# Complex mixing by three real products for two groups at a time, inverse by halves of the array

## The chip, the cores and the metric

The kernel runs on one core of a Trainium2 chip. The metric is the time of one execution on the device in microseconds; the median of three runs before the change is 1173.78 us (1173.12 to 1173.87). The chip has a matrix engine (TensorE: PE for its products, PEld for its weight loads), a vector engine (VectorE, DVE), a scalar engine (ScalarE, ACT), GpSimd (POOL) and a queue engine that only issues transfers (SyncE, SP). They run side by side, each in the order of its own program, and meet at semaphores. Products are written to eight banks of PSUM, of 512 fp32 columns each.

## What is computed

A Fourier layer over a sequence of 3008 tokens (2 sequences, 256 channels), and two feed-forward layers behind it:

```python
X = np.fft.rfft(x, axis=1)
Xr, Xi = (X.real.astype(np.float32), X.imag.astype(np.float32))
Yr = Xr @ w_r - Xi @ w_i + b_r
Yi = Xr @ w_i + Xi @ w_r + b_i
lam = 0.01
Yr = np.sign(Yr) * np.maximum(np.abs(Yr) - lam, 0.0)
Yi = np.sign(Yi) * np.maximum(np.abs(Yi) - lam, 0.0)
y = np.fft.irfft(Yr + 1j * Yi, n=x.shape[1], axis=1)
h = y @ w_in_1;   g = relu(h) + alpha * min(h, 0);            y = g @ w_out_1
h = y @ w_in_2;   g = piecewise quadratic of h;               y = g @ w_out_2
```

The change is in the mixing (the lines of Yr and Yi), in the threshold behind it and in the first step of the inverse transform.

## The kernel before

**The transform.** 3008 is 47 times 64. A first product over 47 points (`real47`, 16 tiles of x) is stored to DRAM and read back in another order (tile `zt`, a quad of four groups, 2 transfers for each quad). Then come 48 steps, one for each group of 64 frequencies (24 groups in each of 2 sequences). A step `s` on TensorE is, in program order: `forward(s)` (the 64-point transform, two fp32 products of 128 columns into `xt_bank[s % 2]`), now and then two late tiles of `real47`, `mix(s - 1)` (12 products of 256 columns into `y_bank`) and `inverse(s - 2)` (one fp32 product of 256 columns into `v_bank`). Two groups share a pair of matrices (`gc`, read from DRAM for each pair) and a pair of results (`v_sb`, stored to DRAM for each pair).

**What the mixing multiplies.** Numbers are split into a high and a low part (f32r), and each product is done as high by high, high by low and low by high. So a step has 2 halves of the channels, 2 parts (real and imaginary) and 3 such terms: 12 products. ScalarE writes the high parts (`split_xt`, L644, L645, the second with the sign turned), VectorE the low parts (L887, L889).

**The threshold** is three operations of VectorE (`threshold`: bias added, L899; clipped, L902; the clipped value taken away, L907). ScalarE's `take_v` (L653) brings the inverse out of PSUM.

**The order around it.** Each engine's order is written out by hand. SyncE's queue holds, for each pair `p` from 3 on: `load_matrices(p)` (L359), for even `p` `load_values(p // 2)` (L370: the quad `zt` that forward of the pair `p` reads), loads of weights (L387, L389), and `store_pair(p - 3)` (L381), which waits for `take_v` of both groups of pair `p - 3`. So the quad that pair `p` reads is issued behind the store of pair `p - 4`. There are two buffers of `zt`.

**Jobs at the end of the transform.** From step 36 on the first tokens of the feed-forward layer are made: `tokens(0, job)` (TensorE, L1187, jobs 0 to 3 at steps 36, 38, 40 and 44), each into the one bank `side_bank`; the next may begin only when ScalarE (`side_copy`, `side_hi`) and VectorE (`side_lo`, `side_t1` and so on) have read the bank (`side_free`). They do that at the end of their steps 37, 39 and 41 to 43.

**The feed-forward layers** (from 153 us on) are products of 376 columns by a seven-product scheme (L1202) and their output products (L1294). The change doesn't touch them.

Of the kernel before, what the change touches and what calls it, by code (L numbers as in the profile page):

```python
# [5 lines left out]
P = 128  # L6
# [27 lines left out]
LATE_TILES = {1: (9,), 3: (10, 11), 5: (12, 13), 7: (14, 15)}  # L34
LATE_STORES = {n: (t, part) for n, (b, part, t) in enumerate(
    (b, part, b * TILES_PER_BATCH + t) for b in range(BATCH) for part in range(1 - b, STORE_PARTS)
    for t in range(0, TILES_PER_BATCH, 2))}
# [5 lines left out]
WAIT_PRODUCTS = {TILES_PER_BATCH - 1: 4 * (512,), TILES_PER_BATCH: 2 * (512,)}  # L43

CLIP_STEPS = WEIGHT_STEP = 21
# [5 lines left out]
SLOTS = 3  # L51

# [19 lines left out]
TOKEN_STEPS = {36: 0, 38: 1, 40: 2, 44: 3}  # L72
# [13 lines left out]
def transform_constants():  # L86
# [39 lines left out]
    both = np.stack([fwd_g, inv_g], axis=2).reshape(GROUPS // 2, 2, P, 2 * P)  # L126
    pairs = both.transpose(0, 2, 1, 3)
    return fwd.astype(np.float32), inv.astype(np.float32), pairs.reshape(GROUPS // 2, P, 4 * P).astype(np.float32)
# [12 lines left out]


def step_pair(s):

    return (s // 2) % SLOTS, (s // 2) // SLOTS


def fft_mix_ffn_kernel(nc, x, wmix, bias, alpha, wpack, fwd47, inv_in, group_consts, out):
# [16 lines left out]
    with ctx:  # L165
# [21 lines left out]
        half = sb("half", [P, 1])  # L187
        ut = [sb(f"ut{i}", [P, TILE_COLS]) for i in range(2)]
# [6 lines left out]
        wm_hi = sb("wm_hi", [P, 4 * D], f32r, fft)  # L195
        wm_lo = sb("wm_lo", [P, 4 * D], f32r, fft)
        bias_sb = sb("bias_sb", [P, D], scope=fft)
        xt_hi = [sb(f"xt_hi{i}", [P, DC, 3 * N2], f32r, fft) for i in range(SLOTS)]
        xt_lo = [sb(f"xt_lo{i}", [P, DC, 3 * N2], f32r, fft) for i in range(SLOTS)]
        y_sum = sb("y_sum", [P, D], scope=fft)  # L200
        y_clip = sb("y_clip", [P, D], scope=fft)
        y_out = [sb(f"y_out{i}", [P, D], scope=fft) for i in range(SLOTS)]
        raw_in_sb = [sb(f"raw_in_sb{i}", [P, (W + 1) * P], scope=fft) for i in range(RAW_SLOTS)]
        raw_out_sb = [sb(f"raw_out_sb{i}", [P, 2 * D], scope=fft) for i in range(RAW_SLOTS)]
        wm_raw = sb("wm_raw", [P, 4 * D], scope=fft)
# [19 lines left out]
        v_bank, xt_bank, y_bank = bank[2], bank[4:6], bank[7]  # L225
        clip_bank = bank[3]
        late_banks = ((bank[0], bank[1]), (bank[3], bank[6]))
# [9 lines left out]
        idle_ready = sem("idle_ready")  # L237
        wm_hi_ready = sem("wm_hi_ready")
# [11 lines left out]
        xt_hi_ready = sem("xt_hi_ready")  # L250
        xt_lo_ready = sem("xt_lo_ready")
        mix_done = sem("mix_done")
        y_sum_ready = sem("y_sum_ready")
        y_clip_ready = sem("y_clip_ready")
# [48 lines left out]
        block = ctx.enter_context(nc.Block())  # L303

# [50 lines left out]
        def _(sp):  # L355
            def load_matrices(p):
                if p >= GC_SLOTS:
                    sp.wait_ge(inv_done, 2 * (p - GC_SLOTS) + 2)
# [24 lines left out]
            def load_weights(n):  # L383
                if n >= RAW_SLOTS:
# [17 lines left out]
            sp.dma_start(wm_raw[:, :], wmix).then_inc(wm_in, 16)  # L402
# [4 lines left out]
            load_x(sp, 9)  # L407
            load_matrices(1)
            load_first_values(1)
            load_x(sp, 10)  # L410
            load_x(sp, 11)
            load_matrices(2)
            load_values(1)
            load_x(sp, 12)
            load_x(sp, 13)
            sp.dma_start(alpha_sb[:, :], alpha).then_inc(const_in, 16)
            sp.dma_start(inv47[:, :], inv_in).then_inc(const_in, 16)
            load_x(sp, 14)
            load_x(sp, 15)

            for p in range(SLOTS, PAIRS):
                load_matrices(p)
                if p % 2 == 0:
                    load_values(p // 2)
                if p == 18:
# [68 lines left out]
        def _(pool):  # L494
# [31 lines left out]
            for s in range(WEIGHT_STEP, STEPS):  # L526
# [7 lines left out]
                if s == 41:  # L534
                    token_lo(0, T1, r[1][:, :])
                if s == 43:
                    token_lo(0, T2, r[0][:, :])
                if s == 45:
# [856 lines left out]
```

## Time and profile before

| | |
|---|---|
| median of 3 runs | 1173.78 us |
| the profiled execution, its own time | 1173.06 us |
| its span, first to last instruction | 1171.3 us |
| TensorE busy | 1161.5 us, 99% of the span |
| VectorE, ScalarE, GpSimd busy | 75%, 73%, 58% |
| TensorE's first product of the layers' output (L1294) | at 153.14 us |
| granted clock of TensorE | 1.00 of full speed |

The span counts from the first to the last instruction; 1.8 us of the profiled execution's own time lie outside it. A busy share is over the whole span. The transform is the first 150 us, and in it each engine's share has to be read by itself.

### The profile page before, as it was taken

What the parts mean: (1) busy time and instruction counts of PE and PEld (TensorE: products, weight loads), DVE (VectorE), ACT (ScalarE), POOL (GpSimd) and SP (SyncE); (2) the same over time, 40 slices, a digit from 0 to 9 for tenths busy, and PEclk for the clock granted to TensorE, in tenths of its full rate; (3) what the DMA queues carried; (4) which work ended last, traced back from release to release, by engine and by line L of the source; (5) the groups of instructions that cost most, each with busy time, mean ns of one, the idle gap of its engine ahead of it and who ended that gap; (6) DMA issues with size and microseconds to landing.
All of it is one profiled execution on the core that took longest, in us unless ns stands there. A gap on an engine that the chain in (4) does not pass through costs nothing.

```text
span 1171.3 us, 21142 instructions
## 1 busy us (share of the span) xinstructions
PE 1161.5 (99%) x7024; PEld 1135.1 (97%) x7024; DVE 882.4 (75%) x1675; ACT 853.7 (73%) x1880; POOL 684.7 (58%) x714
## 2 busy tenths in 40 slices
PE   8999999999999999999999999999999999999998
PEld 3899999999999999999999999999999999999998
DVE  3777777777777777777777787878778787878776
ACT  3445577777676777767677788888888787878776
POOL 0027547567575767666556666665657565756554
PEclk9999999999999999999999999999999999999999
DMA  9898312012120201202004500000000000000000
GB/s 324 312 304 267 123 55 67 29 41 65 49 77 28 68 28 60 77 29 68 19 20 162 197 19 1 27 1 27 1 27 1 28 1 27 2 27 1 14 14 27
DMA packets 41164, 79.56 MB, mean 68 GB/s; under 512 B 4576, under 2 KB 21088, under 8 KB 40288
## 3 DMA queue, kind: packets, MB, share of 16 engines
q1 hardware_dynamic: 38752, 68.65, 17.7%
q10 hardware_dynamic: 2304, 9.56, 2.1%
q8 instruction: 56, 0.92, 0.3%
q14 instruction: 52, 0.43, 0.1%
HBM read 47.92 MB, written 30.28 MB: 67 GB/s over the span
## 4 chain that ended last, share of the span: by engine, by line
PE 98%; DMA 1%; DVE 0%; issue 0%; SPq 0%; ACT 0%; ACTq 0%
PE bank L1294 45%; PE bank L1202 40%; PE bank L1168 6%; PE bank L1187 2%; PE bank L1178 2%; PE bank L1153 2%; DMA x_sb<-x 1%; PE bank L1138 1%; PE bank L1124 0%; DVE g_sb L1004 0%; SPq L339 0%; DVE y_sum L899 0%; DVE a_sb L872 0%; DVE bank L989 0%; DVE y_tile L1026 0%
## 5 line engine op out<-in xcount | busy, mean ns | idle before, releaser
L547 POOL TENSOR_TENSOR g_lo<-g_sb,g_hi 128x376 fp32r<-128x376 f32 x510 | 506.4, 1004 | 361.5 <-ACT g_hi L803 360.7
L1294 PE MATMUL bank<-g_hi,w_out_hi 128*128 128x376 f32 x1024 | 342.8, 335 | 0.0
L1294 PE MATMUL bank<-g_hi,w_out_lo 128*128 128x376 f32 x1024 | 341.5, 333 | 0.0
L1202 PE MATMUL bank<-xc_hi,w_in_hi 128*128 128x376 f32 x896 | 302.4, 338 | 0.1
L1202 PE MATMUL bank<-xc_hi,w_in_lo 128*128 128x376 f32 x896 | 299.6, 334 | 0.0
L1202 PE MATMUL bank<-xc_lo,w_in_hi 128*128 128x376 f32 x896 | 299.0, 334 | 0.0
L803 ACT ACTIVATE g_hi<-g_sb 128x376 fp32r<-128x376 f32 x512 | 261.2, 510 | 45.7 <-DVE g_sb L1004 28.8
L1294 PE MATMUL bank<-g_lo,w_out_hi 128*128 128x376 f32 x1024 | 259.6, 334 | 0.0
L1294 PEld LDWEIGHTS bank<-g_hi,w_out_hi 128*128 128x128 f32 x1024 | 192.2, 188 | 0.6
L1294 PEld LDWEIGHTS bank<-g_hi,w_out_lo 128*128 128x128 f32 x1024 | 192.7, 188 | 0.0
L1294 PEld LDWEIGHTS bank<-g_lo,w_out_hi 128*128 128x128 f32 x1024 | 184.2, 188 | 0.0
L1202 PEld LDWEIGHTS bank<-xc_hi,w_in_hi 128*128 128x128 f32 x896 | 168.3, 188 | 0.8 <-DVE g_sb L1004 0.4
L1202 PEld LDWEIGHTS bank<-xc_hi,w_in_lo 128*128 128x128 f32 x896 | 168.5, 188 | 0.0
L1202 PEld LDWEIGHTS bank<-xc_lo,w_in_hi 128*128 128x128 f32 x896 | 168.4, 188 | 0.0
L792 ACT ACTIVATE act_a<-bank,half 128x376 f32<-128x376 f32 x192 | 109.1, 568 | 43.9 <-PE bank L1202 43.1
L794 ACT ACTIVATE act_a<-act_a 128x376 f32<-128x376 f32 x256 | 133.0, 519 | 8.1
L1004 DVE SCALAR_TENSOR_TENSOR g_sb<-bank,neg_alpha,g_sb 128x376 f32<-128x376 f32 x192 | 115.7, 603 | 3.1 <-ACT bank L788 2.9
L787 ACT ACTIVATE g_sb<-bank 128x376 f32<-128x376 f32 x192 | 91.9, 479 | 34.2 <-PE bank L1202 33.0
L977 DVE TENSOR_TENSOR partial<-u,bank 128x376 f32<-128x376 f32 x128 | 69.5, 543 | 59.9 <-PE bank L1202 58.9
L1008 DVE SCALAR_TENSOR_TENSOR g_sb<-bank,act_a 128x376 f32<-128x376 f32 x192 | 104.6, 545 | 4.8 <-ACT act_a L794 1.2
L984 DVE TENSOR_TENSOR h<-partial,bank 128x376 f32<-128x376 f32 x128 | 69.8, 545 | 41.5 <-PE bank L1202 41.3
L788 ACT ACTIVATE bank<-bank 128x376 f32<-128x376 f32 x192 | 92.1, 479 | 0.0
(84 smaller groups left out, 1511.9 us busy)
## 6 DMA issues: line engine op xcount, KB each, us to landing
gc<-group_consts SPq DMA_DIRECT2D x24, 256.0 KB, 4.4
slots_scratch<-a_sb ACTq DMA_DIRECT2D x24, 256.0 KB, 4.4
inverse_scratch<-v_sb SPq DMA_DIRECT2D x24, 256.0 KB, 3.0
ut<-inverse_scratch SPq DMA_DIRECT2D x16, 384.0 KB, 5.0
out<-y_tile SPq DMA_DIRECT2D x30, 188.0 KB, 1.9
zt<-slots_scratch SPq DMA_DIRECT2D x22, 256.0 KB, 4.1
x_sb<-x SPq DMA_DIRECT2D x10, 512.0 KB, 8.9
prep_raw<-wpack SPq DMA_DIRECT2D x16, 256.0 KB, 2.7
```

The lines of the kernel that those rows point to most:

```text
L547: pool.tensor_tensor(g_lo[kind][:, :], g_sb[n % 3][:, :], g_hi[kind][:, :].bitcast(f32), ALU.subtract)\
L787: act.activation(gg, h, ACT.Relu)
L788: act.activation(h, h, ACT.Relu, scale=-1.0).then_inc(act_done, 1)
L792: act.activation(a, h, ACT.Relu, bias=half[:, 0:1], scale=0.5).then_inc(root_ready, 1)
L794: act.activation(a, a, ACT.Square).then_inc(act_done, 1)
L803: act.activation(g_hi[kind][:, :], g_sb[n % 3][:, :], ACT.Copy).then_inc(hi_ready, 1)
L984: dve.tensor_tensor(h22[:, :], partial[:, :], c12_bank[:, 0:N], ALU.add).then_inc(h_ready[C22], 1)
L1004: dve.scalar_tensor_tensor(out=gg, in0=h_of(kind), scalar=neg_alpha[:, f:f + 1], in1=gg, op0=ALU.mult, op1=ALU.add).then_inc(g_ready, 1)
L1008: dve.scalar_tensor_tensor(out=gg, in0=h_of(kind), scalar=1.0, in1=a, op0=ALU.max, op1=ALU.min).then_inc(g_ready, 1)
L1168: last = pe.matmul(y_bank[:, 0:D], xs[s % SLOTS][:, c, at:at + P], ws[:, (part * DC + c) * D:(part * DC + c + 1) * D], start=n == 0, stop= ...
L1202: done = pe.matmul(bank_of[:, 0:N], w_part[:, fp, w * P:(w + 1) * P], x_part[q % 2][:, xs, :], start=first and n == 0, stop=last_one and n ...
L1294: last = pe.matmul(acc_bank[k][c][:, 0:N], w[:, fp, upper * D + c * P:upper * D + (c + 1) * P], g_part[kind][:, :], start=first and n == 0 ...
```

## The change

Steps become pairs: TensorE runs, for each pair `p`, `forward(p)`, `mix(p - 1)`, `inverse(p - 2)`, one late tile of `real47` (pairs 2 to 8), and a token job (pairs 18 to 21). With A = Xr + Xi, the mixing of both groups is three real products over a stationary operand that holds both groups' values: A by w_r (`X_SUM`, into `sum_bank`), Xi by -(w_r + w_i) (`X_IM`) and Xr by (w_i - w_r) (`X_RE`), both into `parts_bank`. Yr is the first sum and the second, Yi the first and the third. So a pair has 3 products, 2 halves of the channels and 3 terms: 18 products of 256 columns. The sum A is made by VectorE in PSUM from a copy of Xi that ScalarE makes. The threshold is, of y with bias: over = relu(y - lam) on ScalarE and min(y + lam, over) on VectorE. The matrices of the inverse are laid out so that the rows 0 to 63 hold one group and the rows 64 to 127 the other, and the inverse of a pair is four fp32 products of 64 rows each: two for real and imaginary part of each group, one half of the array for each group, into two banks.

```diff
-LATE_TILES = {1: (9,), 3: (10, 11), 5: (12, 13), 7: (14, 15)}
+LATE_TILES = {2: 9, 3: 10, 4: 11, 5: 12, 6: 13, 7: 14, 8: 15}
-WAIT_PRODUCTS = {TILES_PER_BATCH - 1: 4 * (512,), TILES_PER_BATCH: 2 * (512,)}
+WAIT_PRODUCTS = 4 * (512,)
-TOKEN_STEPS = {36: 0, 38: 1, 40: 2, 44: 3}
+TOKEN_PAIRS = {18: 0, 19: 1, 20: 2, 21: 3}
...
@@ TensorE
-            def inverse(s):
-                matrices = gc[s // 2 % GC_SLOTS]
-                pe.wait_ge(y_ready, s + 1)
-                if s:
-                    pe.wait_ge(v_ready, s)
-                pe.matmul(v_bank[:, 0:D], matrices[:, (2 * (s % 2) + 1) * P:(2 * (s % 2) + 2) * P],
-                          y_out[s % SLOTS][:, :], start=True, stop=True).then_inc(inv_done, 1)
+            def inverse(p):
+                matrices = gc[p % GC_SLOTS]
+                pe.wait_ge(y_ready, p + 1)
+                if p:
+                    pe.wait_ge(v_ready, 2 * p)
+                for k in range(2):
+                    for g in range(2):
+                        rows = slice(N2 * g, N2 * (g + 1))
+                        last = pe.matmul(v_bank[g][:, 0:D], matrices[rows, (2 + k) * P:(3 + k) * P],
+                                         y_out[p % MIX_SLOTS][rows, k, :], start=k == 0, stop=k == 1)
+                last.then_inc(inv_done, 1)
+            for p in range(PAIRS):
+                forward(p)
+                if p == PAIRS - 1:
+                    make_p1(0)
+                if p:
+                    mix(p - 1)
+                if p == PAIRS - 1:
+                    side_free(0, 4)
+                    make_p6(0)
+                if p >= 2:
+                    inverse(p - 2)
+                if p in LATE_TILES:
+                    real47(LATE_TILES[p], late_bank, LATE_TILES[p])
+                if p in TOKEN_PAIRS:
+                    tokens(0, TOKEN_PAIRS[p])
@@ ScalarE
+            for p in range(PAIRS):
+                split_x(p)
+                split_sum(p)
+                for s in (2 * p, 2 * p + 1):
+                    weights_hi(s)
+                if p:
+                    over(p - 1)
+                if p == PAIRS - 1:
+                    take_p1(0)
+                if p >= 2:
+                    take_v(p - 2)
+                if p in LATE_TILES:
+                    copy_a(LATE_TILES[p], late_bank[0])
+                for s in (2 * p, 2 * p + 1):
+                    if s in LATE_STORES:
+                        store_a(act, *LATE_STORES[s])
+                if p == 19:
+                    side_copy(0, 0, r[0])
+                    side_hi(0, 0, B11)
+                if p == 20:
+                    side_copy(0, 1, r[2])
@@ VectorE
+            for p in range(PAIRS):
+                split_x(p)
+                sum_x(p)
+                if p:
+                    add_bias(p - 1)
+                    add_parts(p - 1)
+                split_sum(p)
+                if p:
+                    shrink(p - 1)
+                if p in LATE_TILES:
+                    copy_a(LATE_TILES[p], late_bank[1])
+                if p == 19:
+                    side_lo(0, 1, B11)
+                if p == 20:
+                    side_t1(0)
+                if p == 21:
+                    side_t2(0)
+                    side_lo(0, 2, B22)
+                    side_t3(0)
@@ SyncE: load_values keeps its place in the queue, and so does store_pair
-                    sp.wait_ge(b_done, 4 * (n - QUAD_SLOTS) + 4)
+                    sp.wait_ge(b_done, 2 * (n - QUAD_SLOTS) + 2)
```

**The first place: SyncE's queue around the quad of pair 8.** Before, the five transfers are the store of pair 4, the matrices of pair 8, its quad and the store of pair 5:

```order
L381 DMA inverse_scratch<-v_sb1 128x2x256 [waits v_ready]
L359 DMA gc0<-group_consts 128x512 [waits inv_done]
L370 DMA zt0<-slots_scratch2 64x4x256 [waits a_stored02,b_done]
L370 DMA zt0<-slots_scratch2 64x4x256
L381 DMA inverse_scratch<-v_sb2 128x2x256 [waits v_ready]
```

Of the changed kernel, the same stretch:

```order
L406 DMA inverse_scratch<-v_sb1 128x2x256 [waits v_ready]
L384 DMA gc0<-group_consts 128x512 [waits inv_done]
L395 DMA zt0<-slots_scratch2 64x4x256 [waits a_stored02,b_done]
L395 DMA zt0<-slots_scratch2 64x4x256
L406 DMA inverse_scratch<-v_sb2 128x2x256 [waits v_ready]
```

The queue's order is the same. What the store waits for (`v_ready` of pair 4) is what moves: TensorE's inverse of pair 4 was at steps 10 and 11, which is pair 5, and is now in pair 6.

**The second place: ScalarE in the pair 19, and what TensorE does there.** `xt_hi` and `x_im` are the split of the forward transform, `y_over` the threshold, `v_sb` the inverse of pair 17, and `r0` and `xc_hi0` read `side_bank` (bank 1) for the first token job. Before, from step 37 to step 38:

```order
L644 ACTIVATE xt_hi1<-bank5 128x2x128 [waits mix_done,b_done]
L645 ACTIVATE xt_hi1<-bank5 128x2x64
L653 ACTIVATE v_sb2<-bank2 128x256 [waits inv_done]
L662 ACTIVATE w_in_hi<-raw_in_sb2 128x896 [waits s_made]
L679 ACTIVATE r0<-bank1 128x376 [waits side_done]
L672 ACTIVATE xc_hi0<-bank1 128x376 [waits side_done]
L644 ACTIVATE xt_hi2<-bank4 128x2x128 [waits mix_done,b_done]
L645 ACTIVATE xt_hi2<-bank4 128x2x64
```

The changed kernel in pair 19:

```order
L668 ACTIVATE xt_hi1<-bank5 128x2x256 [waits mix_done,b_done]
L672 ACTIVATE x_im<-bank5 128x256 [waits x_sum_ready]
L676 ACTIVATE xt_hi1<-bank5 128x2x128 [waits x_sum_ready]
L704 ACTIVATE w_out_hi<-raw_out_sb2 128x512
L684 ACTIVATE y_over<-bank0,neg_lam 128x512 [waits y_ready,y_sum_ready]
L692 ACTIVATE v_sb2<-bank2 128x256 [waits v_stored2,inv_done]
L692 ACTIVATE v_sb2<-bank7 128x256
L718 ACTIVATE r0<-bank1 128x376 [waits side_done]
L711 ACTIVATE xc_hi0<-bank1 128x376 [waits side_done]
```

The two reads of bank 1 stand now behind `y_over`, which waits for VectorE's sum of this pair's mixing, and behind both halves of `v_sb`.

**The third place: TensorE at the end of the same pair 19**, from the inverse of pair 17 on:

```order
L1262 MATMUL bank2<-y_out1,gc1 128x256 [waits v_ready,y_ready]
L1262 MATMUL bank7<-y_out1,gc1 128x256
L1262 MATMUL bank2<-y_out1,gc1 128x256
L1262 MATMUL bank7<-y_out1,gc1 128x256
L1272 MATMUL bank1<-inv47_sb,ut1 128x94 [waits side_taken,t_made,b_lo_ready,u_in1]
L1272 MATMUL bank1<-inv47_sb,ut1 128x94 x3
L1227 MATMUL bank4<-gc0,zt0 128x2x64 [waits sum_lo_ready,gc_in0,zt_in0]
L1227 MATMUL bank4<-gc0,zt0 128x2x64 x3
```

Before, at step 38 (the first row is the inverse of step 36):

```order
L1178 MATMUL bank2<-y_out0,gc2 128x256 [waits v_ready,y_ready]
L1187 MATMUL bank1<-inv47_sb,ut1 128x94 [waits side_taken,t_made,b_lo_ready,u_in1]
L1187 MATMUL bank1<-inv47_sb,ut1 128x94 x3
L1153 MATMUL bank5<-gc3,zt1 128x128 [waits xt_lo_ready]
L1153 MATMUL bank5<-gc3,zt1 128x128
```

The second token job stood one step behind the step in which the other engines read bank 1 for the first; it stands now at the end of the same pair.

## Rows read from the trace of the kernel before

**Rows 1.** The page: busy time, and the chain that ended last.
```profile
PE 1161.5 (99%) x7024; PEld 1135.1 (97%) x7024; DVE 882.4 (75%) x1675; ACT 853.7 (73%) x1880; POOL 684.7 (58%) x714
PE 98%; DMA 1%; DVE 0%; issue 0%; SPq 0%; ACT 0%; ACTq 0%
```

**Rows 2.** Busy time by stretch: TensorE, VectorE, ScalarE, GpSimd; granted clock, DMA share.
```profile
0.00:20.00 20.00, 15.61 (x76) 4.59 (x76) 7.32 (x12) 7.42 (x12) 0.20 (x4) 1.00 0.89 336
60.00:100.00 40.00, 39.75 (x306) 38.33 (x306) 30.67 (x86) 19.31 (x58) 14.09 (x17) 1.00 0.85 283
```

**Rows 3.** The chain, 34 to 41 us: start, us, what.
```profile
34.74 1.43 PE bank L1168 x12
36.17 0.43 PE bank L1178 x2
36.60 0.44 PE bank L1153 x4
37.05 1.88 PE bank L1138 x16
38.92 1.62 PE bank L1168 x12
```

**Rows 4.** Timeline of TensorE in narrow windows: forward of pairs 0, 8 and 18; first L1294.
```profile
23.40 1.05 PE L1153 MATMUL bank<-gc,zt 128*128 128x128 f32 x8
65.96 0.38 PE L1153 MATMUL bank<-gc,zt 128*128 128x128 f32 x2
113.39 0.38 PE L1153 MATMUL bank<-gc,zt 128*128 128x128 f32 x2
153.14 0.34 PE L1294 MATMUL bank<-g_hi,w_out_hi 128*128 128x376 f32 x1
```

**Rows 5.** ScalarE behind a forward, twice; then groups of both engines by shape.
```profile
24.04 0.38 ACT L644 ACTIVATE xt_hi<-bank 128x256 fp32r<-128x256 f32 x1 [1.76 <-PE bank L1153]
66.78 0.39 ACT L644 ACTIVATE xt_hi<-bank 128x256 fp32r<-128x256 f32 x1 [0.23 <-PE bank L1153]
67.06 0.27 ACT L645 ACTIVATE xt_hi<-bank 128x128 fp32r<-128x128 f32 x1
L617 ACT ACTIVATE a_sb<-bank 128x512 f32<-128x512 f32 x16 | 9.6, 598 | 13.3 <-PE bank L1138 13.3
L880 DVE TENSOR_TENSOR wm_lo<-wm_raw,wm_hi 128x512 fp32r<-128x512 f32 x2 | 1.3, 688 | 1.9 <-ACT wm_hi L636 1.9
L887 DVE TENSOR_TENSOR xt_lo<-bank,xt_hi 128x256 fp32r<-128x256 f32 x48 | 20.3, 423 | 18.7 <-ACT xt_hi L645 17.7
L911 DVE TENSOR_TENSOR xc_lo<-bank,xc_hi 128x376 fp32r<-128x376 f32 x3 | 1.6, 546 | 1.1 <-ACT xc_hi L672 1.1
```

**Rows 6.** SyncE's queue: pair 4's store with the quad of pair 8; then pair 16's.
```profile
57.34 0.38 SPq L381 DMA_DIRECT2D inverse_scratch<-v_sb  x1
58.35 1.41 SPq L370 DMA_DIRECT2D zt<-slots_scratch  x2
113.99 0.38 SPq L381 DMA_DIRECT2D inverse_scratch<-v_sb  x1
```

**Rows 7.** The two issues of each of these quads, and their times to landing.
```profile
L370 SPq DMA_DIRECT2D zt<-slots_scratch x2: 675/684/692, 58.4 to 59.1; - x2
DMA to landing us min/median/max: 4.0/4.9/5.8
L370 SPq DMA_DIRECT2D zt<-slots_scratch x2: 591/604/617, 115.0 to 115.6; - x2
DMA to landing us min/median/max: 3.6/3.9/4.1
```

**Rows 8.** Timeline around the second token job, 120 to 123 us.
```profile
120.54 0.48 ACT L679 ACTIVATE r<-bank 128x376 f32<-128x376 f32 x1
120.90 0.49 ACT L672 ACTIVATE xc_hi<-bank 128x376 fp32r<-128x376 f32 x1
122.08 1.10 PE L1187 MATMUL bank<-inv_sb,ut 96*128 96x94 f32 x8 [0.39 <-issue]
```

More of the change, by code:

```diff
@@ L42 @@
 WARM_PRODUCTS = (512, 256)
[L43 to L45 removed]
+WAIT_PRODUCTS = 4 * (512,)
+WEIGHT_STEP = 21
+BANK_PAIRS = range(10, 21)
 FF = 2048
@@ L51 @@
 SLOTS = 3
+MIX_SLOTS = 2
+X_RE, X_IM, X_SUM = range(3)
 LAYERS = 2
@@ L836, in _ @@
                 prep_high(g)
+                if g == 0:
+                    over(PAIRS - 1)
+                    take_v(PAIRS - 2)
                 if g < ALL_GROUPS:
@@ L1094, in _ @@
                 if g == 0:
-                    threshold(STEPS - 1)
+                    add_bias(PAIRS - 1)
+                    add_parts(PAIRS - 1)
+                    shrink(PAIRS - 1)
                     dve.wait_ge(neg_ready, 1)
@@ L1140, in real47, with forward @@
                     last.then_inc(a_done, 1)
[L1142 to L1144 removed]
+            def forward(p):
+                quad, matrices = p // 2, gc[p % GC_SLOTS]
+                if p == 0:
                     pe.wait_ge(zt_first_in, 32)
[L1146 removed]
+                elif p % 2 == 0 or p == 1:
                     pe.wait_ge(zt_in[quad % QUAD_SLOTS], 32 * (quad // QUAD_SLOTS) + 32)
[L1148 to L1156 removed]
@@ new lines, in forward, with mix @@
+                for g in range(2):
+                    for c in range(DC):
+                        last = pe.matmul(xt_parts(p)[:, c, :, g, :],
+                                         zt[quad % QUAD_SLOTS][:, 2 * (p % 2) + g, c * P:(c + 1) * P],
+                                         matrices[:, g * P:(g + 1) * P], start=True, stop=True)
+                last.then_inc(b_done, 1)
+            def mix(p):
+                slot = p % MIX_SLOTS
+                for n, k in enumerate((X_IM, X_SUM, X_RE)):
+                    if p == 0:
+                        pe.wait_ge(wm_lo_ready, n + 1)
+                    if k == X_IM:
+                        pe.wait_ge(xt_lo_ready, p + 1)
+                        if p:
+                            pe.wait_ge(y_sum_ready, p)
+                    if k == X_SUM:
+                        pe.wait_ge(sum_lo_ready, p + 1)
+                    to = {X_IM: parts_bank[:, 0:D], X_SUM: sum_bank[:, 0:D], X_RE: parts_bank[:, D:]}[k]
+                    terms = [(c, xs, ws) for c in range(DC)
+                             for xs, ws in ((xt_hi, wm_hi), (xt_hi, wm_lo), (xt_lo, wm_hi))]
+                    for n, (c, xs, ws) in enumerate(terms):
+                        last = pe.matmul(to, xs[slot][:, c, k, :], ws[:, k, c * D:(c + 1) * D],
+                                         start=n == 0, stop=n == len(terms) - 1)
+                    if k == X_SUM:
+                        last.then_inc(sum_done, 1)
+                last.then_inc(mix_done, 1)
```

315 lines of the change are left out of this document (151 added, 164 removed).

## The prediction

> **What bounds the kernel now.** I read the page first: TensorE is busy 99% of the span and is 98% of the chain that ended last [rows 1]. A busy share is no proof by itself, so I read the transform by stretches: from 60 to 100 us TensorE works 39.75 of 40 us, VectorE 30.7 and ScalarE 19.3 [rows 2]. TensorE bounds each step, and the others have slack. The chain in order of time gives a step's parts: 12 mixing products 1.43 us (0.119 each), the inverse 0.43, the forward products 0.44, a step of 2.30 [rows 3]. Two late tiles take 1.88 us, and the mixing behind them 1.62 instead of 1.43. What the change does to time is then a question of two sums: how much of TensorE's work goes, and whether TensorE still finds its inputs ready. For the second I read SyncE's queue and how early each transfer lands.
>
> **The work that goes.** A pair has 18 mixing products for 24: 6 x 0.119 = 0.71 us, 17.1 us over 24 pairs. Two idle products go too (0.9 us, but they filled a wait). The forward products keep their columns.
>
> **The inverse by halves.** For a pair it is four fp32 products of 256 columns in place of two. If two halves run side by side, it takes the time of two, 0.86 us, as now. If they take turns, 1.72. The trace has no product of 64 by 128, but it has 64 by 64: sixteen records of 512 columns in 1.88 us [rows 3]. A record of the inverse with 256 columns takes 0.43 / 2 = 0.215 us; sixteen records of 512 in turn would take 16 x 0.43 = 6.9 us. So four run at a time, in both halves of the rows. I take side by side, and keep 0.86 us a pair for the range. There is a price for changing the array's shape: the two late tiles need 4 x 0.43 = 1.72 us and took 1.88, and the mixing behind took 0.19 more: 0.35 us for going in and out. Every pair goes in and out once now: 24 x 0.35 = 8.4 us, against four times before (1.4), and 7 more changes of shape between the inverse and a late tile (1.2). So TensorE's work falls by 17.1 + 0.9 - 8.4 + 1.4 - 1.2 = 9.8 us, and a pair without extras takes 0.88 + 2.14 + 0.86 + 0.35 = 4.2 us for 4.6 now. The Trainium skill, page "TensorEngine Tiling (Array Packing)", section "Tiling Modes", says that tiles work independently and that a change of the tiling mode drains TensorE; the 0.35 us agree with the second, and a sum without it would be 8.2 us better.
>
> **What a pair is waited for: the quad of `zt`.** The queue's order is unchanged: the quad that pair p reads is issued behind the store of pair p - 4, which waits for `take_v` of that pair. But the inverse of a pair now comes two pairs behind its forward, where it came two steps (one pair) behind. So the same transfers start a pair later while the reader stands where it stood. Today the slack is small: the store of pair 4 is issued at 57.34 [rows 6], the second half of the quad at 59.1 and it lands 5.8 us later [rows 7], at 64.9; the forward of pair 8 reads it at 65.96 [rows 4]. From store to landing: 7.6 us there, and 1.6 + 4.1 = 5.7 us for the store at 113.99 [rows 6, 7], when fewer transfers are under way. Moved by 4.2 us or more, the quad comes too late for each even pair.
>
> How long is the loop from one such forward to the next? From rows of the operations nearest in shape, counted from the forward's start:
> - ScalarE starts 0.64 us after four records of forward began (23.40 to 24.04) [rows 4, 5]; a pair has eight, so at 1.07. Its 512 columns take 0.60 [rows 5], and an independent operation starts 0.11 before the end of the last (66.78 and 0.39, then 67.06): `x_im` starts at 1.56 and ends at 1.95.
> - VectorE, 0.04 between dependent operations: low part 512 columns 0.69 to 2.68; `sum_x` 0.42 to 3.14; `add_bias` and `add_parts`, 0.69 each, start 0.08 before the last one's end: the second runs 3.67 to 4.36. The mixing of the pair before ended at 0.88 + 2.14 + 0.2 = 3.2, in time.
> - ScalarE: `over` from 4.40, 0.60; both `take_v` 0.39 each, to 5.56. The inverse has ended by then (4.2 + 0.2).
> - SyncE: the store at 5.6, and the next quad lands 5.7 to 7.6 later. Forward of pair p + 2 starts 11.3 to 13.2 us after that of pair p; now it is 9.2.
>
> I take 12.7 while late tiles and their stores load the DMA engines (they are busy 85% there [rows 2]) and 11.6 behind them. TensorE's wait is 2.5 to 3.5 us in each second pair. It is almost independent of what TensorE's own work costs: the loop doesn't pass through the inverse. That is why the saving of 0.4 us a pair is not added: it goes into the wait.
>
> **The token jobs.** Job 1 on TensorE now stands at the end of pair 19, and ScalarE and VectorE read bank 1 for job 0 only at the end of their own pair 19, behind `over` and `take_v`. Counted as above: `take_v` ends at 5.56, two reads of bank 1 (0.48, 0.49 [rows 8]) to 6.4, VectorE's low part 0.55 [rows 5] to 7.0. TensorE is there at 4.2 and waits 2.9 us; today it waits 0.39 [rows 8]. Job 2 waits for one read and one operation, some 2.7 us; job 3 for three operations of VectorE, 3.5. Pairs 18 to 22 take 5.1 + 8.0 + 7.6 + 8.3 = 29.0 us; a late quad hides behind these waits.
>
> **The sum, as a timeline of forward.** It starts at about 22.2 (23.40 now, for the two idle products less and the first values landing). The second half of the first quad is issued a transfer earlier, so pair 1 follows at 24.2. Then the pair's chain is bare: the mixing of pair 0 waits for VectorE's sum (0.6 us), that of pair 1 for the sum of pair 0 (1.2): pair 2 at 28.2, its store of pair 0 at 28.2 + 5.6 + 1.2 + 0.9 (two issues of ScalarE) = 35.9, the quad 7 us later: pair 4 at 43. Pair 10: 43 + 3 x 12.7 = 81. Pair 18: 81 + 4 x 11.6 = 127.5, for 113.39 now [rows 4]. Pair 22: 156.5. Pair 23: 160.7. From there to the first product of L1294 TensorE has forward 0.88, two mixings 4.28, three inverses 3.63, nine products of the layer at 3 x 0.119 x 376 / 256 = 0.52, 4.7, and one wait of 0.8 for the sum: 14.3 us. That is 175.0, for 153.14 now [rows 4]: **21.9 us later**. Nothing behind it changes, and TensorE is full there, so the end moves by the same. The profiled execution took 1173.06 us with a span of 1171.3; its span becomes 1193.2 and its time 1195.0. The median shown is 0.7 us above it, so I predict **1195.5 us**.
>
> **Rivals.**
> - *The quads arrive in time, and TensorE's own work decides* (0.05). It needs store to landing under 2 x 4.2 - 5.6 = 2.8 us; the two cases above are 5.7 and 7.6. Then pairs without late tiles take 4.2, those with one 5.2: pair 18 comes at 28 + 7 x 5.3 + 9 x 4.2 = 103; with 29.0 and 4.2 + 14.3 the first L1294 is at 150.5, 2.6 us earlier than now: 1171 us. This is the case on the other side.
> - *The halves take turns* (0.10). 0.86 us a pair more, of which the wait for the quad absorbs nearly all: `take_v` moves from 4.9 to 5.2, so 0.3 for each of 7 loops, 2.6 for the last three inverses, 1.5 at the start: 6 us more, 1201.5.
> - *The clock falls in the waits* (0.08). The longest stretches without work so far are at the start, where TensorE works 15.6 of 20 us and the granted clock stays 1.00 [rows 2]. Waits of 3 us in each second pair are new; if TensorE went to its lower level (1.2 in place of 2.4 GHz), the forward and mixing behind a wait, which do stand in the loop, would take up to 3 us more in up to ten loops: 1205 to 1225. The Trainium skill, page "TensorE: Matmul & The Clock Gate", section on why it matters for kernels, warns of idle gaps between bursts of products; no row here shows such a fall.
> - *The same mechanism, with lighter traffic* (0.09). With longer pairs there is less traffic, and if all quads took 5.0 us the loop would be 10.6: 7 loops save 1.0 to 2.1 each, 1186 or a little below.
>
> **How the numbers follow.** The forecast with its own range of 1187 to 1204 has 0.68. The range reaches down to the light traffic and up over halves in turn: 1185 to 1206, which leaves out the first rival and the clock. A measurement of this kernel can tell 0.2% (2.3 us) from no change. Slower: 0.94; the first rival splits into same (0.03) and faster (0.03).
>
> **What would show it.** In the changed profile: SyncE's store behind `take_v` and the quad landing just before forward of each even pair from 4 on; TensorE idle 2.5 to 3.5 us there, released by the transfer into `zt`; three waits of 2.7 to 3.5 us before L1272 in pairs 19 to 21; inverse records of both halves starting together, 0.86 us for a pair; 2.14 us for a pair's mixing; granted clock 1.00. The prediction is wrong if the wait before even pairs is under 1 us, if it is ScalarE's or VectorE's (the loop would then be longer in every pair), or if the clock falls.

## The result and the profile after the change

The changed kernel takes **1211.46 us** (median of 4 runs, 1208.11 to 1216.50), the kernel before 1173.49 (4 runs): ratio 1.033, 95% interval 1.029 to 1.037, so 38.0 us more where 22 more were forecast, and above the range. The four runs spread over 8.4 us, those of every other kernel here over 0.8 to 5.5 us; so a difference from this median of 1211.46 is known to some 5 us only. Two executions that ran at a granted clock of 0.75 all through (1399 us, the profiled one of e5_takes_early, and 1409 us, the kernel before) count in no comparison. The profiled execution is the longest of them: 1216.50 us, span 1214.7.

The page of the changed kernel first (L1227 is the forward, L1247 the mixing, L1262 the inverse, L1272 the token jobs, L1379 the output products; L1294 of the forecast is now L1379):

```profile
span 1214.7 us, 20878 instructions
PE 1169.0 (96%) x6972; PEld 1132.7 (93%) x6972; DVE 879.5 (72%) x1583; ACT 869.4 (72%) x1881; POOL 683.2 (56%) x714
PE   7877779999999999999999999999999999999998
PEclk8888889999999999999999999999999999999999
```

The reader is to see that nearly all the loss lies in the first six slices of 30 us, the transform (the first output product comes 42.1 us later than before, the end 43.4): there TensorE's busy digit falls to 7 and 8, and so does its granted clock, which the forecast had at 1.00. What TensorE waited for, in the view of its waits (us in total, times, longest):

```profile
PE bank L1227 <- DMA zt<-slots_scratch: 26.9, 10, 4.7
PE bank L1272 <- DVE xc_lo L981: 3.0, 1, 3.0
PE bank L1272 <- DVE r L998: 3.0, 1, 3.0
PE bank L1272 <- DVE r L989: 2.5, 1, 2.5
PE bank L1227 <- DMA gc<-group_consts: 0.8, 2, 0.5
```

These are the waits that were forecast, at the places that were forecast: `zt` before the forward of each even pair from 4 to 18, and three token jobs (2.9, 2.7 and 3.5 forecast). Two of the ten for `zt`, 1.1 and 1.4 us, stand before pairs 0 and 1. The other eight are 1.8 to 4.7 us long, 3.0 in the mean, where 2.5 to 3.5 was forecast. The stretches of 20 us answer to [rows 2] (TensorE's busy time in the second number, its granted clock third from the end):

```profile
20.00:40.00 20.00, 16.30 (x110) 13.64 (x110) 10.32 (x19) 7.60 (x17) 0.00 (x0) 0.83 0.75 261
60.00:80.00 20.00, 16.02 (x106) 13.21 (x107) 10.08 (x17) 8.12 (x20) 0.00 (x0) 0.83 0.67 234
80.00:100.00 20.00, 15.79 (x124) 12.73 (x122) 13.07 (x24) 10.00 (x23) 2.41 (x5) 1.00 0.68 225
140.00:160.00 20.00, 15.65 (x96) 14.60 (x97) 7.50 (x13) 7.56 (x17) 6.96 (x11) 0.76 0.59 183
```

A mean of 0.83 is a mixture of two levels, which short stretches behind a wait show apart:

```profile
35.00:42.00 7.00, 7.00 (x58) 4.78 (x58) 5.79 (x11) 3.28 (x8) 0.00 (x0) 1.00 0.53 167
46.00:51.00 5.00, 5.00 (x23) 5.00 (x24) 1.45 (x3) 1.25 (x3) 0.00 (x0) 0.50 0.86 334
63.00:68.00 5.00, 5.00 (x25) 4.84 (x23) 1.81 (x3) 1.25 (x3) 0.00 (x0) 0.50 0.62 214
82.00:87.00 5.00, 5.00 (x42) 3.79 (x34) 2.96 (x6) 2.82 (x7) 0.00 (x0) 1.00 0.64 210
```

From 46 to 51 us, right behind the wait for the quad of pair 4, TensorE is busy without a gap and gets 23 matmul records through; from 82 to 87 us 42. The one stretch is at 1.2 GHz, the other at 2.4. Single instructions show the same: a mixing product that starts each 0.12 us at full clock starts each 0.21 here.

```profile
41.27 1.09 PE L1212 MATMUL bank<-x_sb,fwd_sb 64*64 64x512 f32 x8
46.00 2.08 PE L1227 MATMUL bank<-gc,zt 128*128 128x128 f32 x8 [3.65 <-DMA zt<-slots_scratch]
48.09 0.41 PE L1247 MATMUL bank<-wm_lo,xt_hi 128*128 128x256 f32 x1
48.30 0.42 PE L1247 MATMUL bank<-wm_hi,xt_lo 128*128 128x256 f32 x1
...
51.23 0.28 PE L1247 MATMUL bank<-wm_lo,xt_hi 128*128 128x256 f32 x1
51.34 0.28 PE L1247 MATMUL bank<-wm_hi,xt_lo 128*128 128x256 f32 x1
```

The transform has eight such stretches, 41 us together; the first begins at 24 us, at the start, the other seven in or just behind one of the waits above. At most half of that, 20 us, is lost, less where the slower work lies in a wait.

The forward of pairs 0, 4, 10, 18, 22 and 23 starts at 23.3, 46.0, 89.9, 141.4, 176.3 and 180.6 us (forecast 22.2, 43, 81, 127.5, 156.5 and 160.7; before, [rows 4]), and the first output product at 195.2 (forecast 175.0).

One loop of the forecast, ScalarE, SyncE's queue and TensorE from 95 us on:

```profile
95.20 0.64 ACT L692 ACTIVATE v_sb<-bank 128x256 f32<-128x256 f32 x2
95.86 0.38 SPq L406 DMA_DIRECT2D inverse_scratch<-v_sb  x1
96.28 1.36 SPq L384 DMA_DIRECT2D gc<-group_consts  x1
97.74 1.25 SPq L395 DMA_DIRECT2D zt<-slots_scratch  x2
102.49 0.80 PE L1227 MATMUL bank<-gc,zt 128*128 128x128 f32 x2 [3.36 <-DMA zt<-slots_scratch]
```

The forward of pair 10 started at 89.91. `take_v` of its turn ends at 95.84, the store goes out at 95.86, 5.95 us behind the forward (5.6 forecast), the quad behind it is read at 102.49, 6.6 us later (5.7 to 7.6 forecast), and TensorE has waited 3.4 us.

### The profile page after: what moved, and what is told of

It is laid out like the page before. It is cut to its first block, busy times and chain, and to the rows that moved or that the text cites. A ratio compares the mean times of both kernels' runs of the same rounds, so it can differ in the third digit from the quotient of the medians.

```text
span 1214.7 us, 20878 instructions
## 1 busy us (share of the span) xinstructions
PE 1169.0 (96%) x6972; PEld 1132.7 (93%) x6972; DVE 879.5 (72%) x1583; ACT 869.4 (72%) x1881; POOL 683.2 (56%) x714
## 3 DMA queue, kind: packets, MB, share of 16 engines
q1 hardware_dynamic: 38752, 68.78, 17.1%
## 4 chain that ended last, share of the span: by engine, by line
PE 64%; DVE 0%; issue 0%
PE bank L1379 34%; PE bank L1287 29%; PE bank L1272 1%; DVE u L1044 0%; DVE y_tile L1098 0%
## 5 line engine op out<-in xcount | busy, mean ns | idle before, releaser
L1379 PE MATMUL bank<-g_hi,w_out_lo 128*128 128x376 f32 x1024 | 342.9, 335 | 0.0
L1379 PE MATMUL bank<-g_hi,w_out_hi 128*128 128x376 f32 x1024 | 342.4, 334 | 0.0
L1379 PE MATMUL bank<-g_lo,w_out_hi 128*128 128x376 f32 x1024 | 259.8, 335 | 0.0
L1379 PEld LDWEIGHTS bank<-g_hi,w_out_hi 128*128 128x128 f32 x1024 | 192.5, 188 | 0.8
L1379 PEld LDWEIGHTS bank<-g_hi,w_out_lo 128*128 128x128 f32 x1024 | 192.4, 188 | 0.0
L1379 PEld LDWEIGHTS bank<-g_lo,w_out_hi 128*128 128x128 f32 x1024 | 184.7, 188 | 0.0
```

The lines of the kernel that those rows point to most:

```text
L1379: last = pe.matmul(acc_bank[k][c][:, 0:N], w[:, fp, upper * D + c * P:upper * D + (c + 1) * P], g_part[kind][:, :], start=first and n == 0 ...
```

## The experiments

Each ratio is to the kernel before, timed on the same chip (its median was 1173.57 beside e1 to e4, 1174.47 beside e5 to e8, 1173.82 beside e9 to e11, 1174.35 beside e12); a difference between kernels of two of these groups carries that of the chips, up to 0.9 us.

**e1_quads_early** takes the quads' lateness away: SyncE issues the quad an iteration earlier, ahead of the store, and the store ahead of the late tile's x.

```diff
                 load_matrices(p)
-                if p % 2 == 0:
-                    load_values(p // 2)
+                if p % 2 and p + 1 < PAIRS:
+                    load_values((p + 1) // 2)
+                if p > SLOTS:
+                    store_pair(p - SLOTS - 1)
                 if p + 8 < TILES:
                     load_x(sp, p + 8)
...
-                store_pair(p - SLOTS)
```

> The changed kernel with one edit in SyncE's queue: the quad of pair p + 1 and the matrices of pair p are issued ahead of the store of pair p - 4, not behind it. Theory A (the waits for the quads, those of the token jobs, and a clock that falls in such waits): the ten waits for zt (26.9 us) go, and with them most falls of the clock; left are the three token waits (one of them longer, since a late quad no longer hides in it) and waits of 0.5 to 1 us per pair for VectorE's sum, because ScalarE's chain of a pair is 4.5 us and more. Time 1184 us (1179 to 1190). Rival B (the loop of ScalarE and VectorE is what limits a pair, the quad only happens to be last): the other waits take the place of these, 1200 us or more. Rival C (the clock falls for another reason, the 64-row products for one): still 6 to 8 falls, 1200 us.

Measured: 1193.66 us, ratio 1.017 (1.015 to 1.019), 17.8 us under the changed kernel and between theory A (1179 to 1190) and its rivals (1200). So the late quads, with what the clock does in their waits, were 17.8 of the 38 us. The wait for `zt` is 1.8 us in all, and other waits are longest:

```profile
PE bank L1273 <- DVE xc_lo L982: 4.5, 1, 4.5
PE bank L1273 <- DVE r L999: 3.6, 1, 3.6
PE bank L1228 <- issue: 3.5, 2, 3.0
PE bank L1248 <- DVE bank L969: 2.7, 4, 1.0
```

The token jobs' waits have grown, and the clock still fell four times, two of them there (120 to 140 us: 0.83, 140 to 160: 0.91).

**e2_quads_reads** is e1_quads_early and, on ScalarE and VectorE, the reads of bank 1 for the token jobs at the start of the next pair, ahead of that pair's own work.

```diff
 # ScalarE (VectorE alike, with side_lo, side_t1, side_t2, side_t3)
+                if p == 19:
+                    side_copy(0, 0, r[0])
+                    side_hi(0, 0, B11)
+                if p == 20:
+                    side_copy(0, 1, r[2])
...
-                if p == 19:
-                    side_copy(0, 0, r[0])
-                    side_hi(0, 0, B11)
```

> e1 with one more edit: ScalarE's and VectorE's reads of bank 1 for a token job stand at the start of the next pair, ahead of its split, not at the end behind y_over and v_sb. Theory A: the three token waits (8.5 us) nearly go, clock 1.00 throughout; ring waits for VectorE's sum remain. Time 1177 us (1173 to 1182), about 7 to 8 us below e1. Rival B: 1192 or more. Rival: VectorE is delayed by the reads at the start of the pair and gives the same back at the mixing: no better than e1.

Measured: 1181.25 us, ratio 1.007 (1.005 to 1.008): another 12.4 us, inside theory A's 1173 to 1182. **e9_reads_early**, run later, is the fourth corner: the reads moved by the same edit, the quads late as in the changed kernel.

> The changed kernel with its quads issued as they are, and only ScalarE's and VectorE's reads of bank 1 for token jobs 0 to 3 moved to the start of the pair that follows (so before that pair's own work instead of behind the pair's before). Theory A (the loop through the quad of zt sets the pace also in pairs 18 to 22, and the token waits lie beside it): 1 to 4 us off, 1209 (1206 to 1212). Theory B (the three token waits of 2.5 to 3.0 us stand in the sum on their own, and with them go two stretches at the half clock): 10 us off, 1201 (1198 to 1204).

Measured: 1197.36 us (1195.05 to 1200.38), ratio 1.020 (1.018 to 1.022), 14.1 below the changed kernel: theory A falls, and theory B's 1198 to 1204 is missed by a little. The token jobs' waits are gone, the quads' stay:

```profile
PE bank L1230 <- DMA zt<-slots_scratch: 23.6, 12, 4.0
```

Pairs 18 to 22 take 24.3 us for 34.9. So the four kernels read 1211.5 (neither), 1193.7 (quads), 1197.4 (reads), 1181.3 (both): the effects, 17.8 and 14.1, add up to the 30.2 of both within the spread of the runs. Two separate causes make four fifths of the loss; what the clock does in their waits is inside both.

How far one execution stands for a kernel shows here too. Up to pair 18 the program of e9_reads_early is that of the changed kernel, and its profiled execution is there at 130.96 us, the changed kernel's at 141.38. In the same 718 records of TensorE the one had a mean clock of 0.95, the other of 0.90:

```profile
0.00:130.70 130.70, 102.64 (x718) 76.93 (x718) 74.56 (x130) 61.62 (x134) 25.39 (x34) 0.95 0.76 256
0.00:141.00 141.00, 109.25 (x718) 81.72 (x718) 74.68 (x130) 61.93 (x134) 26.18 (x36) 0.90 0.71 237
```

**e3_fill_waits** asks what the clock costs: all waits stay, idle products stand in them (results unused), nine of 512 columns before the forward of the even pairs from 4 to 18, ten before token jobs 1 to 3.

```diff
+            def filler(p, n):
+                pe.wait_ge(sum_lo_ready, p - 1)
+                for _ in range(n):
+                    pe.matmul(xt_bank[p % 2][:, 0:512], wm_hi[:, 0, 0:P], wm_hi[:, 1, 0:512],
+                              start=True, stop=True)
...
+                if p >= 4 and p % 2 == 0 and p - 1 not in (19, 21):
+                    filler(p, 9)
```

> The changed kernel with products of no use (512 columns, f32r) ahead of the forward of the even pairs from 4 (9 products, 2.1 us) and ahead of token jobs 1 to 3 (10 products, 2.4 us), written to the bank that the next forward overwrites. All waits stay as late as they are, but TensorE works in them. If the waits make the clock fall (theory A): granted clock 1.00, and 1195 us (1191 to 1199), 16 us less than the changed kernel, which is the time that the late quads and tokens cost by themselves. If the clock falls for another reason: 1211 us and falls as before.

Measured: 1204.05 us (1203.29 to 1205.52), ratio 1.026 (1.025 to 1.028), between the two expectations (1195 and 1211). More work on TensorE, and 7.4 us less time: the reader should stop at that. All four runs lie below the changed kernel's fastest, 1208.11; by the spread of both, the 7.4 can be some 5 us more or less. Two stretches at the lower level are left, 10.2 us together, at 23.0 and 108.3 us:

```profile
20.00:40.00 20.00, 17.03 (x114) 14.22 (x116) 10.58 (x19) 7.61 (x17) 0.00 (x0) 0.83 0.76 265
40.00:60.00 20.00, 19.98 (x144) 14.97 (x140) 12.52 (x24) 9.04 (x21) 0.00 (x0) 1.00 0.92 310
```

They can cost 5.1 us at most. So of the 38 us the clock has 7.4 to 12.5, and without it the changed kernel would take 1199 to 1204. One run says more: the fastest of the four, 1203.29 us, had a mean granted clock of 1.000, so no such stretch, and is 0.8 us under the median. The clock's share is then near 8 us, and what the two stretches cost near 1. The idle products themselves hardly delay the quads: seven of the eight quads landed 0.04 to 0.05 us before the forward that reads them, the one of pair 6 half a microsecond before.

**e8_fill_all** was to close that gap: 13 and 12 products in place of 9 and 10, and four float32 products behind the ninth tile.

> The changed kernel with all its waits, and idle products in them: 13 before the forward of an even pair in place of the 9 of e3_fill_waits, 12 in place of 10 before the token jobs, and four more of 512 columns behind the ninth tile at the start. Theory A (the clock took about 10 us of the 38, the waits 28): the granted clock is 1.00 all through, the time 1200 us (1197 to 1203). Theory B (the idle products themselves delay the forward where they are longer than the wait): the clock is 1.00 and the time 1204 or more.

Measured: 1207.58 us, ratio 1.028 (1.027 to 1.030): theory B. The clock is 1.00 outside 20 to 40 us, and 1.000 in three of the four runs (1206.62 to 1207.94), but the products were longer than the waits. A float32 product of 512 columns is two records of 0.43 us, so the four take 3.4 us of the start at the full clock, and more where it is halved. It leaves the clock's share as it is.

**e4_before_late_quad** puts the suspected cost alone into the kernel before: its quad is issued behind the store of pair p - 3 instead of p - 4.

```diff
-                if p % 2 == 0:
-                    load_values(p // 2)
...
                 store_pair(p - SLOTS)
+                if p % 2 == 0:
+                    load_values(p // 2)
```

> The kernel before with one edit: each quad is issued behind the store of pair p - 3, one place later in SyncE's queue; all mixing, thresholds and inverses as before. Theory A: waits of 0.7 to 1.3 us for zt before each even pair from 6 or 8 on, 7 us in all, too short for the clock to fall: 1180.5 us (1177 to 1186). If a late quad costs nothing by itself (its wait hides another): 1173.5.

Measured: 1180.92 us, ratio 1.006 (1.005 to 1.008), as theory A has it. The view of waits gives `zt` six times, at most 1.9 us, and the clock is 1.00 in all stretches of 20 us from 20 to 160:

```profile
PE bank L1153 <- DMA zt<-slots_scratch: 5.4, 6, 1.9
120.00:140.00 20.00, 18.80 (x149) 18.16 (x150) 13.39 (x36) 10.86 (x31) 11.74 (x14) 1.00 0.53 171
```

The lateness of the quad alone costs 7.4 us with the old order of the inverse and waits under 2 us; with the new one, whose loop is longer, 17.8.

**e5_takes_early** goes on from e2_quads_reads, which is still 7.7 us above before. ScalarE's reads of the inverse's bank go into the time in which it waits for VectorE.

```diff
                 split_x(p)
+                if p >= 3:
+                    take_v(p - 3)
                 split_sum(p)
...
-                if p >= 2:
+                if p == PAIRS - 1:
                     take_v(p - 2)
```

> The kernel of the run before (quads issued early, token reads at the start of a pair) with one more move: ScalarE's two reads of the inverse's bank (take_v) for pair p - 3 go from behind `over` to between the split of pair p and the split of its sum, where ScalarE has waited for VectorE. Theory A (with the quads in time, what is left of the 1181.2 us is a ring of ScalarE and VectorE: ScalarE's work behind `over`, 0.8 us, delays the next pair's split, and so the sum that TensorE's next mixing needs): pairs 4 to 18 fall from 4.9 to about 4.4 us and the time to 1170 us (1167 to 1174). Theory B (the pair is TensorE's own work plus late tiles, and the store now goes a little later): the time stays at 1181 (1179 to 1184).

Measured: 1177.41 us, ratio 1.0030 (1.0017 to 1.0043): 3.8 us less, between the two theories. No row of its profile is read.

**e6_full_rows** and **e7_four_products** price the two halves of the change itself in this stream. Both also have the second `weights_hi` behind `over`; that operation is ScalarE's, not VectorE's as both expectations say. In the first the inverse is two products of 128 rows, which leaves out the separation of the two groups; in the second the X_RE terms are issued twice, and that product comes out doubled.

```diff
-                    for g in range(2):
-                        rows = slice(N2 * g, N2 * (g + 1))
-                        last = pe.matmul(v_bank[g][:, 0:D], matrices[rows, (2 + k) * P:(3 + k) * P],
-                                         y_out[p % MIX_SLOTS][rows, k, :], start=k == 0, stop=k == 1)
+                    last = pe.matmul(v_bank[k][:, 0:D], matrices[:, (2 + k) * P:(3 + k) * P],
+                                     y_out[p % MIX_SLOTS][:, k, :], start=True, stop=True)
```
```diff
+                    if k == X_RE:
+                        terms = terms + terms
```

> The kernel of e5_takes_early, with the shrinking operation of VectorE for the second weight moved behind `over` (0 to 1 us), and the inverse as two products of all 128 rows in place of four of 64: the number of changes of the array's shape falls by two a pair, and the separation of a pair's two groups is left out, so the values are not the reference's. Theory A of the prediction's sum (0.35 us for going in and out of the half shape): TensorE's work falls by 8 us; where TensorE bounds all pairs the time is 8 us under e5_takes_early, where other waits take it up it is 1 to 3 us. Theory B (the change of shape is free in a stream that waits anyway): within 1 us.

> The kernel of e5_takes_early (with that same small move of VectorE) with the six terms of the product X_RE issued twice: 24 mixing products for each pair, as many as before the change; that product then comes out doubled. It prices the three-product form by itself. Theory A (TensorE bounds the pairs now that the waits are gone): 24 x 0.71 = 17 us above e5_takes_early, of which up to 4 us hide in waits that are left: +13 to +17. Theory B (other engines' ring bounds them): +5 or less.

Measured: e6_full_rows 1176.39 us, ratio 1.0017 (1.0008 to 1.0026), 1.0 less than e5_takes_early; e7_four_products 1186.22, ratio 1.010 (1.009 to 1.011), 8.8 more. The six products are worth some 8.8 of their 17.1 us here, give or take the small move: neither 13 nor 5. In e7_four_products TensorE is the bound and the others' waits are covered:

```profile
60.00:160.00 100.00, 99.12 (x789) 86.69 (x787) 67.46 (x119) 61.13 (x136) 44.71 (x52) 1.00 0.65 213
```

For e6_full_rows the whole says little: 1 us fits the lower end of theory A and theory B alike, and what took up the rest is not shown. A pair without extras says it better. TensorE in e10_matrices_early (below), halves:

```profile
83.91 0.36 PE L1255 MATMUL bank<-wm_hi,xt_hi 128*128 128x256 f32 x1
86.24 1.13 PE L1270 MATMUL bank<-y_out,gc 64*128 64x256 f32 x8
87.31 0.94 PE L1235 MATMUL bank<-gc,zt 128*128 128x128 f32 x6
```

and in e6_full_rows, full rows:

```profile
101.79 0.36 PE L1253 MATMUL bank<-wm_hi,xt_hi 128*128 128x256 f32 x1
104.02 1.03 PE L1266 MATMUL bank<-y_out,gc 128*128 128x256 f32 x4
104.89 1.05 PE L1233 MATMUL bank<-gc,zt 128*128 128x128 f32 x8
```

From start to start the mixing takes 2.33 for 2.23 us and the inverse 1.07 for 0.87: going in and out of the half shape costs 0.30 us (0.35 in the sum). Eight records of 256 columns in 1.07 us also settle that the halves run side by side: in turn they would take 8 x 0.215 = 1.72.

**e10_matrices_early** takes up the next wait, 3.3 us before the forward of pair 4, for which the profile shows no releaser. In e6_full_rows the matrices of pair 4 are issued at 36.8 us and land 7.2 us later, at 44.0, and the forward starts at 44.10 (the second and third row are of the matrices of pairs 4 and 5):

```profile
44.10 1.13 PE L1233 MATMUL bank<-gc,zt 128*128 128x128 f32 x8 [3.30 <-issue]
L384 SPq DMA_DIRECT2D gc<-group_consts x2: 430/676/923, 36.8 to 39.8; - x2
DMA to landing us min/median/max: 7.2/7.6/8.0
```

The edit is a fifth buffer for the matrices, each issued a pair earlier and so ahead of the late tile's 512 KB.

```diff
-GC_SLOTS = 4
+GC_SLOTS = 5
...
             load_matrices(2)
+            load_matrices(3)
             load_x(sp, 10)
...
-                load_matrices(p)
+                if p + 1 < PAIRS:
+                    load_matrices(p + 1)
```

> The kernel of e6_full_rows with the inverse by halves again (the reference's values), a fifth buffer for a pair's matrices, and each pair's matrices issued one pair earlier, ahead of the late tile's x, which is the last 0.5 MB ahead of them in SyncE's queue. Theory A (the 3.3 us before the forward of pair 4, for which no releaser is shown, and 1.0 us elsewhere are the matrices landing late): 4 to 6 us below e5_takes_early's 1177.4, 1172 (1170 to 1175). Theory B (the 3.3 us are the quad's second half, landing at the same time, or late tiles then come later by as much): 1176 to 1179.

Measured: 1171.17 us (1170.48 to 1171.58, 9 runs), ratio **0.9975** (0.9966 to 0.9985): theory A. This version, which leaves nothing out, beats both kernels: 40.3 us under the changed one and 2.7 under the one before. TensorE is nearly full again where it was not, from 60 to 130 us:

```profile
60.00:130.00 70.00, 67.56 (x535) 58.70 (x535) 53.01 (x94) 47.22 (x109) 36.79 (x45) 1.00 0.83 268
```

**e11_start_filled** and **e12_start_fitted** ask what is left in the start, where a wait of 1.9 us for `zt` before pair 2 has the clock at its lower level from 30 to 34 us behind it.

```diff
 # e12_start_fitted
             for p in range(PAIRS):
+                if p == 1:
+                    idle_products((512,), 1)
+                if p == 2:
+                    pe.wait_ge(sum_lo_ready, 1)
+                    for _ in range(7):
+                        pe.matmul(xt_bank[0][:, 0:512], wm_hi[:, 0, 0:P], wm_hi[:, 1, 0:512],
+                                  start=True, stop=True)
                 forward(p)
```

> The kernel of e10_matrices_early with idle products in the two waits at the start of the transform: four of 512 columns behind the ninth tile and six before the forward of pair 1. Theory A (the clock falls once or twice at 20 to 50 us, because of the waits there, and gives back 2 to 4 us if it doesn't): granted clock 1.00 all through, 1169 (1167 to 1172), below before's 1173.5 to 1174.5. Theory B (the half clock falls into stretches that wait anyway): within 1 us of e10_matrices_early.

> The kernel of e10_matrices_early (1171.2) with idle products cut to its two waits at the start: one float32 product (two records of 0.43 us) before the forward of pair 1, which waited 1.25 us, and seven products of 512 columns in one record of 0.21 us before that of pair 2, which waited 1.91 us. Theory A (the stretch of half clock at 30.1 to 33.8 us comes from these waits, and the mixing of 18 products in it stands on TensorE's path): clock 1.00 all through, 1.5 us less, 1169.6 (1168.6 to 1170.6). Theory B (it is taken up by waits that follow, or the products are in the way as in e11_start_filled): 1171 or more.

Measured: e11_start_filled 1175.20 us, ratio 1.0010 (1.0001 to 1.0019), and e12_start_fitted 1171.15, ratio 0.9973 (0.9963 to 0.9983). The first is 4 us slower than e10_matrices_early, which neither of its theories has: its float32 products don't fit the waits. The idle ones (L1206) stand for 10.7 us in its timeline, in part at the half clock:

```profile
22.65 5.40 PE L1206 MATMUL bank<-a_sb 128*128 128x512 f32 x8
27.89 1.05 PE L1235 MATMUL bank<-gc,zt 128*128 128x128 f32 x8
28.78 5.32 PE L1206 MATMUL bank<-a_sb 128*128 128x512 f32 x12
```

The second is as fast as e10_matrices_early, theory B. The stretch at 30 us is gone from its profile, but there the ninth tile's x came 2.7 us late and the clock fell behind that wait instead. The runs settle what one such stretch at the start is worth: four of the nine had a mean granted clock of 1.000 and took 1169.83 to 1171.81 us, the other five 1170.26 to 1171.91. These runs can't tell that it costs anything.

```profile
21.41 1.18 PE L1220 MATMUL bank<-x_sb,fwd_sb 64*64 64x512 f32 x8 [2.65 <-DMA x_sb<-x]
22.89 2.08 PE L1235 MATMUL bank<-gc,zt 128*128 128x128 f32 x8 [0.30 <-DMA zt<-slots_scratch]
```

## Why the forecast was right and where it failed

- **TensorE's work.** The sum held. A pair without extras takes 4.32 us in e10_matrices_early (4.2 forecast), the halves run side by side, the shape costs 0.30 us (0.35).
- **The quad's loop.** The mechanism held: the waits stand before the even pairs from 4 on, released by the transfer. The size was short in two terms, and this is the second half of the miss. Forward to store is 5.9 us at full clock (5.6). And store to landing doesn't get lighter behind pair 10: 6.6, 5.7, 5.7 and 7.7 us for the stores behind the forwards of pairs 10, 12, 14 and 16, 6.4 in the mean, where 6.0 was taken; the last has the tokens' own loads behind it. With the waits filled (e3_fill_waits) pairs 4 to 18 take 89.6 us, at most 1.7 of it from the clock, for the 84.5 forecast.
- **The token jobs.** Right in place, 3.0, 2.5 and 3.0 us for 2.9, 2.7 and 3.5; pairs 18 to 22 take 34.9 for 29.0 us, with 12.2 us of it at the lower level. Taking the waits away gives 10.6 us there and not 8.5, since most of the clock's part goes with them; the other 3.5 of the 14.1 are within the spread of the runs.
- **The clock.** This is the step that failed. The rival "the clock falls in the waits" had a chance of 0.08 and the line "granted clock 1.00" stood among the signs, and the sum had no term for it, on the ground that the longest stretches without work of before, at the start, left it at 1.00. But no single wait among those was over 1.7 us, and the new ones were forecast at 2.5 to 3.5, so the ground did not reach them. The longest of before is this one:

```profile
PE bank L1138 <- DMA x_sb<-x: 2.3, 3, 1.7
```

The clock fell in eight stretches, and e3_fill_waits shows that this costs 7.4 to 12.5 us, near 8 by its run at 1.000. The rival's price, up to 3 us in each of ten loops, was of the right kind: a loop with its forward at the lower level took forward to store 7.7 us (pair 4, 46.00 to 53.68) and 8.0 (pair 6), for 5.9. The result lies inside the rival's 1205 to 1225. The Trainium skill's warning, page "TensorE: Matmul & The Clock Gate", section on why it matters for kernels, of idle gaps between bursts of products was quoted and then outweighed by a single stretch of rows. The trace of the changed kernel agrees with the warning: the clock fell in or behind seven of its eleven waits for `zt` and before token jobs from pair 4 on.
- **The sum of it.** 1211.5 is 16.0 over the forecast: 7.4 to 12.5 the clock (about 8), the remaining 3.5 to 8.6 (about 8) the loop's and the waits' terms. In e3_fill_waits the first output product comes at 183.1 us, 8.1 over the forecast's 175.0: 1.1 up to pair 4, 5.1 in pairs 4 to 18, 1.5 in pairs 18 to 22 and 0.4 behind them. Without the clock the time would have lain inside the forecast's range, so it is the clock that took it out.
- **Two small slips in the sum.** Its own terms give 1195.7 us (1195.0 and 0.7), not 1195.5; and the first rival takes 5.2 us for a pair with a late tile and adds up with 5.3. Neither matters here.

Not shown is why ScalarE's earlier `take_v` gave 3.8 us and not 11. Of e10_matrices_early's 6.2 us against e5_takes_early the matrices have most: e6_full_rows has ScalarE's small move too, and e10_matrices_early is 5.2 us under it (4.9 by the ratios, since the chips differ) although it goes back to the half shape.

## What to carry to other kernels

A change that makes a stage one step later moves everything that is issued behind its result; count the loop from the reader through the store to the next load before counting the work saved, since here two reorderings of queues (quads ahead of stores, reads of a bank at the start of a step) decided 30 us and the saved products 9. Where a forecast has new waits of two or three microseconds that recur on TensorE, price them twice, with the clock kept and with the work behind each wait at half the clock, and give the second case a real chance. A quick test of it is to fill the waits with products whose results nobody reads, shorter than the wait: if time falls, the clock was part of it. And where the profile names no releaser of a wait, look up when the transfers that the engine needs have landed.

## What the runs showed of the hardware

- More work on TensorE made the kernel faster: 7.4 us by idle products in its waits (e3_fill_waits).
- A wait is no sure sign. In the changed kernel the clock was at 1.2 GHz in or behind waits of 4.66, 3.65, 3.36, 3.20, 2.97, 2.52 and 2.46 us, and stayed at 2.4 behind others of 2.96, 2.87, 2.38 and 1.76; in e10_matrices_early it fell behind one of 1.91, in e4_before_late_quad it stayed behind one of 1.92.
- The kernel with most of these falls has the widest spread: 8.4 us between the four runs of the changed kernel (mean clock 0.983 to 0.987), 1.1 between the nine of e10_matrices_early (0.997 to 0.999). Falls alone don't make a spread: the four runs of e1_quads_early, at 0.991 and 0.992, lie within 1.0 us.
- Products of the two row halves start 6 to 7 ns apart in the records (86.229 and 86.235 us in the changed kernel), and share the time of one.
